# Linear attention, expert MLP and dense MLP on one Trainium2 core: clearing, weight order, late tiles and the last group rearranged

## The chip, the cores and the metric

The kernel runs on one core of one Trainium2 chip. The metric is the device time of one execution in microseconds (us); the median of three executions of the kernel before is 473.36 us (473.33 to 474.61). A difference of 0.3% or less, 1.4 us, can't be told from no change.

## What is computed

The reference, cut to what matters:

```python
def attn(q, k, v, alpha):            # B=2, H=8, S=768, D=48
    for t in range(S):
        state = alpha[:, :, t, :, None] * state + einsum('bhd,bhe->bhde', k[:, :, t], v[:, :, t])
        y[:, :, t] = einsum('bhd,bhde->bhe', q[:, :, t], state)

def moe(x, w_gate, w1, w2, capacity=384):   # x 1536x384, E=8, F=1024
    logits = x @ w_gate; e = argmax(logits); gate_w = softmax(logits)[e]
    # token i goes to the next free slot of expert e, if fewer than capacity are taken
    h = relu(disp @ w1[e]); y = h @ w2[e]
    out[i] = gate_w[i] * y[e, pos[i]]        # 0 where the token was dropped

def mlp(x, w_in, w_out):                     # 384 -> 2048 -> 384
    h = x @ w_in
    return (h * clip(h + 3, 0, 6) / 6) @ w_out

out = mlp(moe(attn(q, k, v, alpha)))
```

## The kernel before

The kernel has three stages, and each engine has its own instruction list, written out by hand; semaphores alone set the order between engines.

**Attention and routing.** The 1536 tokens are 12 tiles of 128. The `for i in range(NT)` loops of the VectorE, ScalarE and TensorE programs (lines 870, 599 and 1112) go through the tiles one by one. For tile `i`, VectorE prepares the decays of tile `i + 3` (`prepare`, five instructions), masks the scores of tile `i + 1` (`mask`) and adds to the state (`update_state`); TensorE computes scores (`front`), state updates (`update`), the carried part (`carry`), the masked part (`mix`), and for the tile before the router's logits (`turn_x`, `logits`); ScalarE copies results out of PSUM. Routing is done in parts, groups of tiles: `PARTS` (line 40) has tiles 0 to 5, 6 to 8, 9, and 10 with 11. For each part, `choose` finds the expert of each token on VectorE, TensorE counts ranks with one-hots (`ranks_before`, `ranks_within`), `exponents` on ScalarE and `weigh` on VectorE give the gates, `place_tokens` the slots. `gate_rows` on ScalarE then scales a token's row by its gate, and GpSimd scatters it to its slot in DRAM with an indirect DMA (line 502). The last part (`LATE`, tiles 10 and 11) is used for the first expert without waiting for that: `gather_first_rows` (line 1147) reads expert 0's rows back from DRAM, transposes them (line 1153, 12 matmuls against the identity), and adds the late tiles by matmuls against one-hots scaled by the gate (line 1159, `to_slots`, six for each late tile).

**Experts.** All weights and inputs are split into a high and a low part (float32r), and three matmuls make a product. `expert(e, r, half)` (line 1203) runs 8 hidden blocks `f` of 9 matmuls and, three blocks behind (`LAG`), 8 output blocks of 9; at `f` = 3, 4 and 6 (`TURN_AT`) it transposes a third of the next expert's rows (line 1166). At `f` = 0, 3, 5 and 7 (`SPLIT_AT`) ScalarE and VectorE split the four pieces of the next expert's weights, raw -> `w_hi` (line 640) -> `w_lo` (line 848). `raw` has one buffer for each piece, so SyncE issues piece `n` of the stage after next when that split is done (`load_piece`, line 331). SyncE's order is: the rows of expert `e + 2`, then its four weight pieces (`during`, line 414). Ahead of the loop stand the loads for expert 2 and one DMA that zeroes the whole output (line 422). GpSimd, once expert 0's rows are turned, clears `x_hi` and `x_lo` (lines 509 and 510), the input of the MLP; ScalarE and VectorE wait for that ahead of expert 1. VectorE works out the offsets of the experts' tokens in that input (lines 933 to 940) between the low parts of expert 0's rows (line 917) and its own part of expert 0.

**MLP.** The weights w_in and w_out are stages 8 and 9. Four groups of three token tiles go through `group` (line 1308): 16 hidden blocks (lines 1174 to 1176) and, three behind, 16 output blocks (lines 1302 to 1304) of nine matmuls of 384 columns. ScalarE copies the three tiles of a group out (line 706), and GpSimd scatters each to its tokens (line 525). A conditional pass (`n_more > 0`) handles experts with more than 232 tokens.

Of the kernel before, what the change touches and what calls it, by code (L numbers as in the profile page):

```python
# [16 lines left out]
def build_program(nc, qk, alpha, v, w_gate, w1, w2, w_in, w_out, out, *, cap):  # L17
# [21 lines left out]

    PARTS = ((0, TPB), (TPB, NT - 3), (NT - 3, NT - 2), (NT - 2, NT))  # L40
    LATE = PARTS[-1]
    NB = E + NG
    FE, FM = F // P, F2 // P
# [11 lines left out]
    with ExitStack() as ctx:  # L55
# [3 lines left out]
        def sem(name):  # L59
            return ctx.enter_context(nc.semaphore(name))  # L60
# [37 lines left out]
        def view(cols):  # L98
            a = arena[0]
            arena[0] += cols  # L100
            assert arena[0] <= ARENA
            return base[:, a:a + cols]
# [13 lines left out]
        rows_at = arena[0]  # L116
        rows = [view(ET * DM) for _ in range(2)]
        routing_at = arena[0]

# [11 lines left out]

        x_late = [base[:, rows_at + (ET + n) * DM:rows_at + (ET + n + 1) * DM] for n in range(2)]
        arena[0] = 0
# [12 lines left out]
        assert arena[0] <= rows_at  # L146
        to_slots = [probs[0][0][:, n * ER:(n + 1) * ER] for n in range(2)]

# [73 lines left out]
        late_gated = sem("late_gated")  # L222
        outputs_zeroed = sem("outputs_zeroed")
        ids_cleared = sem("ids_cleared")
# [110 lines left out]
        def _(sp):  # L335
# [78 lines left out]
            def during(e, r):  # L414

                load_rows(e + 2, r)
                load_stage(e + 2)

            load_rows(2, 0)
            load_stage(2)  # L420

            sp.dma_start(out.rearrange("(c p) d -> p c d", p=P),
                         zrow.rearrange("p (o d) -> p o d", o=1).broadcast_to([P, NT, DM])).then_inc(out_cleared, 16)
            during(1, 1)
            with sp.Fori(1, E // 2 - 1) as t:
# [5 lines left out]
                         allow_slow_non_contiguous=True).then_inc(ids_in, 16)  # L431
            load_stage(E + 1)

            sp.wait_ge(more_end, 1)
# [17 lines left out]
        def _(pool):  # L452
# [54 lines left out]

            pool.wait_ge(rows_turned, KC)
            pool.memset(x_hi[:, :].bitcast(F32), 0.0).then_inc(outputs_zeroed, 1)
            pool.memset(x_lo[:, :].bitcast(F32), 0.0).then_inc(outputs_zeroed, 1)  # L510

# [22 lines left out]
        def _(act):  # L534
# [64 lines left out]
            for i in range(NT):  # L599
                if i == 8:  # L600
                    exponents(0)
                if i == 10:
                    exponents(1)
                if i + 1 < NT:
                    copy_keys(i + 1)
                if i >= 1:
                    copy_xT(i - 1)
                if i + 1 < NT:
                    spread_values(i + 1)
                    scale_state(i + 1)  # L610
                if i == 9:
                    gate_rows(0, (3, 4, 5))
                if i == 10:
                    gate_rows(1, (6,))
                if i == 11:
                    gate_rows(1, (8,))
                    gate_rows(2, (9,))
                if i >= 1:
                    copy_logits(i - 1)
                if 4 <= i < 4 + NPC:  # L620
                    split_first(i - 4)
                copy_x(i)
                if i == 8:
                    gate_rows(0, (0, 1, 2))
                if i == 10:
                    exponents(2)
                    gate_rows(1, (7,))
            copy_xT(NT - 1)
# [41 lines left out]
            act.wait_ge(offsets_ready, 1)  # L670
            act.wait_ge(outputs_zeroed, 2)
            expert(1, 1)
# [53 lines left out]
        def _(dve):  # L726
# [108 lines left out]
            def place_late():  # L835

                a, b = LATE
                dve.wait_ge(late_placed, 1)
                dve.wait_ge(gates_ready, len(PARTS))
                dve.wait_ge(mixed, NT - 1)  # L840
                for i in range(a, b):
                    dve.tensor_scalar(to_slots[i - a], slot_numbers, place[:, i:i + 1], gate[:, i:i + 1],
                                      ALU.is_equal, ALU.mult).then_inc(to_slots_ready, 1)
                dve.tensor_copy(slot[:, a:b], place[:, a:b]).then_inc(slots_ready, 1)
# [25 lines left out]
            for i in range(NT):  # L870
                if i + 1 < NT:
                    mask(i + 1)
                update_state(i)
                if i == 8:
                    place_tokens(0)
                    weigh(0)
                if i == 9:
                    split_lo(0, 0, 0)
                    choose(1)
                if i == 10:  # L880
                    weigh(1)
                    place_tokens(1)
                    choose(2)
                    split_lo(0, 0, 1)
                if i == 11:
                    weigh(2)
                    place_tokens(2)
                    split_lo(0, 0, 2)
                    split_lo(0, 0, 3)
                if i + 3 < NT:  # L890
                    prepare(i + 3)
                if i == 7:
                    choose(0)
            choose(3)
            weigh(3)
# [60 lines left out]
            dve.wait_ge(offsets_ready, 1)  # L956
            dve.wait_ge(outputs_zeroed, 2)
            expert(1, 1)
# [9 lines left out]
            with dve.If(n_more > 0):  # L968
                with dve.Fori(0, n_more) as m:
# [11 lines left out]
                    last.then_inc(more_lo, 1)  # L981

                    e = which(m)
                    at = dve.value_load(offsets[0:1, bass.ds(e, 1)], min_val=0, max_val=NT * P - EN - 1)
                    dve.wait_ge(more_hi, m * 4 + 4)
# [3 lines left out]
                    last.then_inc(more_lo, 1)  # L989
                    dve.wait_ge(more_lo, m * 4 + 4)  # L990
                    for c in range(KC):
# [27 lines left out]
        def _(pe):  # L1019
# [92 lines left out]
            for i in range(NT):  # L1112
                if i + 1 < NT:
                    front(i + 1)
                if i >= 1:
                    turn_x(i - 1)
                if i == 8:
                    pe.wait_ge(const_ready, 4)
                    pe.wait_ge(state_updated, updates_to(i - 1))
                    ranks_within(0)  # L1120
                if i == 9:
                    pe.wait_ge(ranks_read, 1)
                if i == 10:
                    pe.wait_ge(state_updated, updates_to(i - 1))
                    ranks_before(1)
                    ranks_within(1)
                if i == 11:
                    pe.wait_ge(state_updated, updates_to(i - 1))
                    pe.wait_ge(ranks_read, 2)
                    ranks_before(2)  # L1130
                    ranks_within(2)
                update(i)
                carry(i)
                if i >= 1:
                    logits(i - 1)
                mix(i)
# [66 lines left out]
            def expert(e, r, half):  # L1203


                first = isinstance(e, int) and e == 0
                pe.wait_ge(xt_lo_ready, e * KC + KC)
                for f in range(FE):
                    if f % 4 == 0:
                        pe.wait_ge(w_lo_ready, e * NPC + f // 4 + 1)  # L1210
                    hidden(e * FE, f, r)
                    g = f - LAG
                    if g < 0 and not first:
                        outputs(e - 1, FE + g, 1 - r)
                    if g >= 0:
                        if g % 4 == 0:
                            pe.wait_ge(w_lo_ready, e * NPC + 2 + g // 4 + 1)
                        outputs(e, g, r)
                    if half is not None and f in TURN_AT:
                        if f == TURN_AT[0]:  # L1220
                            pe.wait_ge(rows_in[1 - r], half)
                        turn_rows(e + 1, 1 - r, TURN_AT.index(f))
# [13 lines left out]
            with pe.If(n_more > 0):  # L1236
                pe.wait_ge(y_lo_ready, E * KC)
                with pe.Fori(0, n_more) as m:
# [7 lines left out]
                    last.then_inc(more_turned, 1)  # L1246
                    pe.wait_ge(more_lo, m * 4 + 2)
                    for f in range(FE):
# [8 lines left out]
                    last.then_inc(more_hidden, 1)  # L1257
                    pe.wait_ge(more_lo, m * 4 + 3)
                    for c in range(KC):
# [32 lines left out]

            def mlp_outputs(g, f):
                pe.wait_ge(hid_lo_ready, E * FE + g * FM + f + 1)
                o = (f % 4) * DM
                hi, lo = (x[1][:, f // 4, o:o + DM] for x in (w_hi, w_lo))
                for t in range(TT):
                    if f == 0 and g >= 1:
# [9 lines left out]
            def group(g):  # L1308
                for f in range(FM + LAG):
                    if f < FM and not (g == 0 and f < LAG):  # L1310
# [10 lines left out]
            for g in range(NG):  # L1321
                group(g)


# [20 lines left out]
```

## Time and profile before

| | |
|---|---|
| median of three executions | 473.36 us |
| the profiled execution | 473.34 us |
| its span | 471.5 us |
| TensorE busy | 426.0 us |
| VectorE, ScalarE, GpSimd busy | 268.2, 211.1, 61.8 us |
| mean granted TensorE clock | 0.967 |
| attention and routing | 0 to about 97 us |
| gather of expert 0's rows, experts | about 97 to 257 us |
| MLP | about 260 to 463 us |

PE is TensorE, DVE VectorE, ACT ScalarE, POOL GpSimd, SP SyncE. A group of instructions is named by its line, what it writes and what it reads. The number after "x" is a count. The granted clock is the share of TensorE's full clock.

### The profile page before, as it was taken

Reading aid. Unit: us, or ns where it says so; the run is one execution under the profiler, and the core shown is the slowest. Engines: PE = TensorE matmul, PEld = TensorE weight load, DVE = VectorE, ACT = ScalarE, POOL = GpSimd, SP = SyncE. Lnnn points to the kernel's source line nnn. Section 1 sums busy time; section 2 is a strip of 40 time slices with the busy share of each in tenths; the row PEclk is TensorE's granted clock in tenths of the full one; section 3 lists DMA queues with packets and bytes.
Section 4 is the critical chain, followed back from the end, with each engine's and each line's share of the span. In section 5 each row is a group of like instructions: output and inputs, shape, how many; then the busy total and the mean of one; then the engine's idle time right before and its main releaser. Section 6 shows DMA issues by size and latency. Waiting matters only on the chain.

```text
span 471.5 us, 8025 instructions
## 1 busy us (share of the span) xinstructions
PE 426.0 (90%) x3111; PEld 419.6 (89%) x3111; DVE 268.2 (57%) x473; ACT 211.1 (45%) x408; POOL 61.8 (13%) x68
## 2 busy tenths in 40 slices
PE   1899989765998599999998999999999999999992
PEld 1799989655998599999998999999999999999992
DVE  7999998849654466776667365333332433243330
ACT  1255666412652456556565354343333433343331
POOL 8000006538720000000000000020002000020002
PEclk9999999967999599999999999999999999999998
DMA  8999943561699856666575100010000000010001
GB/s 178 297 281 299 297 126 111 193 239 36 134 126 307 299 165 218 221 202 232 153 235 160 60 1 0 1 51 1 0 1 33 18 1 1 0 51 1 0 1 50
DMA packets 37923, 56.36 MB, mean 120 GB/s; under 512 B 4768, under 2 KB 27808, under 8 KB 37888
## 3 DMA queue, kind: packets, MB, share of 16 engines
q1 hardware_dynamic: 35840, 50.95, 37.7%
q0 software_dynamic: 1920, 4.73, 2.6%
q8 instruction: 24, 0.39, 0.4%
q10 hardware_dynamic: 128, 0.20, 0.2%
q14 instruction: 11, 0.09, 0.1%
HBM read 44.06 MB, written 11.81 MB: 118 GB/s over the span
## 4 chain that ended last, share of the span: by engine, by line
PE 70%; DVE 12%; DMA 6%; issue 5%; ACT 3%; SPq 1%; POOL 1%; DVEq 0%; ACTq 0%; POOLq 0%
PE bank L1176 11%; PE bank L1175 11%; PE bank L1174 11%; PE bank L1304 7%; PE bank L1303 7%; PE bank L1302 7%; PE bank L1195 4%; PE bank L1197 4%; PE bank L1196 4%; DMA raw<-w 3%; DVE bwd L743 2%; DVE arena L756 2%; DVE offsets L935 2%; DVE arena L772 1%; DMA arena<-v 1%
## 5 line engine op out<-in xcount | busy, mean ns | idle before, releaser
L848 DVE TENSOR_TENSOR w_lo<-raw,w_hi 128x1536 fp32r<-128x1536 f32 x40 | 70.1, 1757 | 33.5 <-ACT w_hi L640 33.5
L1004 DVE SCALAR_TENSOR_TENSOR arena<-arena,bank 128x384 f32<-128x384 f32 x64 | 35.4, 553 | 83.6 <-ACT arena L712 83.6
L712 ACT ACTIVATE arena<-bank,bias 128x384 f32<-128x384 f32 x64 | 37.0, 578 | 68.5 <-PE bank L1176 68.5
L1174 PE MATMUL bank<-x_hi,w_hi 128*128 128x384 f32 x192 | 64.5, 336 | 2.5 <-issue 2.5
L1195 PE MATMUL bank<-hid_hi,w_hi 128*128 128x232 f32 x192 | 54.4, 283 | 12.7 <-DVE x_lo L925 7.7
L1175 PE MATMUL bank<-x_lo,w_hi 128*128 128x384 f32 x192 | 65.1, 339 | 0.0
L1303 PE MATMUL bank<-w_lo,hid_hi 128*128 128x384 f32 x192 | 64.8, 337 | 0.0
L1176 PE MATMUL bank<-x_hi,w_lo 128*128 128x384 f32 x192 | 64.7, 337 | 0.0
L1304 PE MATMUL bank<-w_hi,hid_lo 128*128 128x384 f32 x192 | 64.7, 337 | 0.0
L1302 PE MATMUL bank<-w_hi,hid_hi 128*128 128x384 f32 x192 | 64.6, 336 | 0.0
L640 ACT ACTIVATE w_hi<-raw 128x1536 fp32r<-128x1536 f32 x36 | 53.2, 1479 | 9.8 <-DMA raw<-w 9.8
L1008 DVE SCALAR_TENSOR_TENSOR hid_lo<-arena,hid_hi 128x384 fp32r<-128x384 f32 x64 | 35.8, 559 | 37.9 <-ACT hid_hi L715 37.9
L1174 PE MATMUL bank<-xt_hi,w_hi 128*128 128x232 f32 x192 | 55.5, 289 | 1.0 <-DVE xt_lo L917 0.9
L1197 PE MATMUL bank<-hid_lo,w_hi 128*128 128x232 f32 x192 | 53.9, 281 | 0.0
L525 POOL DMA_INDIRECT out<-arena,token_at x12 | 11.7, 975 | 321.1 <-ACT arena L706 318.7
L1176 PE MATMUL bank<-xt_hi,w_lo 128*128 128x232 f32 x192 | 53.7, 280 | 0.0
L1196 PE MATMUL bank<-hid_hi,w_lo 128*128 128x232 f32 x192 | 53.7, 280 | 0.0
L1175 PE MATMUL bank<-xt_lo,w_hi 128*128 128x232 f32 x192 | 53.4, 278 | 0.0
L715 ACT ACTIVATE hid_hi<-arena 128x384 fp32r<-128x384 f32 x64 | 33.6, 526 | 43.0 <-DVE arena L1004 39.9
L1195 PEld LDWEIGHTS bank<-hid_hi,w_hi 128*128 128x128 f32 x192 | 38.0, 198 | 13.3 <-DVE x_lo L925 7.5
L1174 PEld LDWEIGHTS bank<-xt_hi,w_hi 128*128 128x128 f32 x192 | 37.6, 196 | 1.6 <-DVE xt_lo L917 1.3
L1197 PEld LDWEIGHTS bank<-hid_lo,w_hi 128*128 128x128 f32 x192 | 37.9, 198 | 0.0
(137 smaller groups left out, 815.2 us busy)
## 6 DMA issues: line engine op xcount, KB each, us to landing
raw<-w SPq DMA_DIRECT2D x32, 768.0 KB, 6.1
slots_x<-arena SPq DMA_DIRECT2D x8, 576.0 KB, 5.7
arena<-qk SPq DMA_DIRECT2D x22, 192.0 KB, 4.4
arena<-slots_x SPq DMA_DIRECT2D x8, 384.0 KB, 4.9
raw<-w_in SPq DMA_DIRECT2D x4, 768.0 KB, 4.5
raw<-w_out SPq DMA_DIRECT2D x4, 768.0 KB, 6.4
arena<-alpha SPq DMA_DIRECT2D x24, 96.0 KB, 3.6
arena<-v SPq DMA_DIRECT2D x12, 192.0 KB, 4.7
```

The lines of the kernel that those rows point to most:

```text
L640: act.activation(w_hi[w][:, n, :], raw[:, n, :], ACT.Copy).then_inc(w_hi_ready, 1)
L712: act.activation(shifted[f % 2], hidden_bank[f % NH][:, 0:BR], ACT.Relu, bias=bias3[:, 0:1]).then_inc(shift_ready, 1)
L848: dve.tensor_tensor(w_lo[w][:, n, :], raw[:, n, :], w_hi[w][:, n, :].bitcast(F32), ALU.subtract)\
L1174: pe.matmul(bank_, hi, hi_in, start=(kc == 0), stop=False)
L1175: pe.matmul(bank_, hi, lo_in, start=False, stop=False)
L1176: return pe.matmul(bank_, lo, hi_in, start=False, stop=(kc == KC - 1))
L1195: pe.matmul(bank_, hi, h_hi, start=(f == 0), stop=False)
L1196: pe.matmul(bank_, lo, h_hi, start=False, stop=False)
L1197: last = pe.matmul(bank_, hi, h_lo, start=False, stop=(f == FE - 1))
L1302: pe.matmul(bank_, h_hi, hi, start=(f == 0), stop=False)
L1303: pe.matmul(bank_, h_hi, lo, start=False, stop=False)
L1304: last = pe.matmul(bank_, h_lo, hi, start=False, stop=(f == FM - 1))
```

## The change

- `PARTS` becomes tiles 0 to 5, 6 and 7, 8, and 9 to 11: three tiles are late. The parts 1 and 2 are handled one tile earlier on VectorE, ScalarE and TensorE, and the first weight split of VectorE (`split_lo(0, 0, 0)`) stands behind `choose(2)`. The late tiles' buffers are put where the attention's `v_apart` and `probs` lie, so `place_late` waits for the last `mix`.
- GpSimd's two clearings and the waits for them go.
- The DMA that zeroes the output moves from ahead of expert 3's rows to behind all weight loads. The rows of expert `e + 2` are loaded ahead of its fourth weight piece in place of ahead of its first.
- In expert 0, TensorE goes through the first three hidden blocks by thirds of the input (`kc` outside), waiting for one third at a time.
- In the last group of the MLP, the last three output blocks are done tile by tile.
- In the conditional pass, the columns behind an expert's own tokens are multiplied with a mask before the addition.

```diff
-    PARTS = ((0, TPB), (TPB, NT - 3), (NT - 3, NT - 2), (NT - 2, NT))
+    PARTS = ((0, TPB), (TPB, NT - 4), (NT - 4, NT - 3), (NT - 3, NT))
     LATE = PARTS[-1]
+    LATE_PART = len(PARTS) - 1
...
+        stays = rows[1][:, 0:MR]
...
-        x_late = [base[:, rows_at + (ET + n) * DM:rows_at + (ET + n + 1) * DM] for n in range(2)]
-        to_slots = [probs[0][0][:, n * ER:(n + 1) * ER] for n in range(2)]
+        to_slots = [probs[n // 2][n % 2][:, 0:ER] for n in range(LATE[1] - LATE[0])]
+        x_late = [v_apart[n // 2][:, n % 2 * DM:(n % 2 + 1) * DM] for n in range(LATE[1] - LATE[0])]
...
@@ SyncE
             def during(e, r):
-                load_rows(e + 2, r)
-                load_stage(e + 2)
-            load_rows(2, 0)
-            load_stage(2)
-            sp.dma_start(out.rearrange("(c p) d -> p c d", p=P),
-                         zrow.rearrange("p (o d) -> p o d", o=1).broadcast_to([P, NT, DM])).then_inc(out_cleared, 16)
+                for n, src in enumerate(stage_source(e + 2)):
+                    if n == NPC - 1:
+                        load_rows(e + 2, r)
+                    load_piece(sp, e + 2, n, src)
+            during(0, 0)
             during(1, 1)
...
             load_stage(E + 1)
+            sp.dma_start(out.rearrange("(c p) d -> p c d", p=P),
+                         zrow.rearrange("p (o d) -> p o d", o=1).broadcast_to([P, NT, DM])).then_inc(out_cleared, 16)
@@ GpSimd
-            pool.wait_ge(rows_turned, KC)
-            pool.memset(x_hi[:, :].bitcast(F32), 0.0).then_inc(outputs_zeroed, 1)
-            pool.memset(x_lo[:, :].bitcast(F32), 0.0).then_inc(outputs_zeroed, 1)
@@ ScalarE
-                if i == 8:
-                    exponents(0)
-                if i == 10:
-                    exponents(1)
+                if i >= 8 and i < 8 + LATE_PART:
+                    exponents(i - 8)
                 if i + 1 < NT:
                     copy_keys(i + 1)
...
                 if i == 10:
-                    gate_rows(1, (6,))
-                if i == 11:
-                    gate_rows(1, (8,))
-                    gate_rows(2, (9,))
+                    gate_rows(2, (8,))
...
                 copy_x(i)
-                if i == 10:
-                    exponents(2)
-                    gate_rows(1, (7,))
+                if i == 9:
+                    gate_rows(1, (6, 7))
...
-            act.wait_ge(outputs_zeroed, 2)
@@ VectorE
-                dve.wait_ge(mixed, NT - 1)
+                dve.wait_ge(mixed, NT)
...
                 if i == 9:
-                    split_lo(0, 0, 0)
-                    choose(1)
-                if i == 10:
                     weigh(1)
                     place_tokens(1)
                     choose(2)
+                    split_lo(0, 0, 0)
+                if i == 10:
+                    weigh(2)
+                    place_tokens(2)
                     split_lo(0, 0, 1)
                 if i == 11:
-                    weigh(2)
-                    place_tokens(2)
                     split_lo(0, 0, 2)
                     split_lo(0, 0, 3)
                 if i + 3 < NT:
                     prepare(i + 3)
                 if i == 7:
                     choose(0)
+                if i == 8:
+                    choose(1)
...
-            dve.wait_ge(outputs_zeroed, 2)
...
+                    dve.tensor_scalar(stays, slot_numbers[:, 0:MR], float(EN), kept[:, bass.ds(e, 1)], ALU.add, ALU.is_ge)
@@ TensorE
-                if i == 9:
-                    pe.wait_ge(ranks_read, 1)
-                if i == 10:
-                    pe.wait_ge(state_updated, updates_to(i - 1))
-                    ranks_before(1)
-                    ranks_within(1)
-                if i == 11:
+                if i in (9, 10):
                     pe.wait_ge(state_updated, updates_to(i - 1))
-                    pe.wait_ge(ranks_read, 2)
-                    ranks_before(2)
-                    ranks_within(2)
+                    pe.wait_ge(ranks_read, i - 8)
+                    ranks_before(i - 8)
+                    ranks_within(i - 8)
...
                 first = isinstance(e, int) and e == 0
-                pe.wait_ge(xt_lo_ready, e * KC + KC)
+                if first:
+                    pe.wait_ge(w_lo_ready, 1)
+                    for kc in range(KC):
+                        pe.wait_ge(xt_lo_ready, kc + 1)
+                        for f in range(LAG):
+                            last = hidden_part(f, kc, 0, xt_hi[0][:, kc * EN:(kc + 1) * EN],
+                                               xt_lo[0][:, kc * EN:(kc + 1) * EN], EN)
+                            if kc == KC - 1:
+                                last.then_inc(hidden_done, 1)
+                else:
+                    pe.wait_ge(xt_lo_ready, e * KC + KC)
...
             def group(g):
-                for f in range(FM + LAG):
+                for f in range(FM + (LAG if g < NG - 1 else 0)):
...
             for g in range(NG):
                 group(g)
+            for t in range(TT):
+                for f in range(FM - LAG, FM):
+                    mlp_outputs(NG - 1, f, (t,))
```

## Rows read from the trace of the kernel before

**Rows 1.** The page, part 1: busy us, share of the span, instructions of each engine.

```profile
PE 426.0 (90%) x3111; PEld 419.6 (89%) x3111; DVE 268.2 (57%) x473; ACT 211.1 (45%) x408; POOL 61.8 (13%) x68
```

**Rows 2.** Waits of PE: engine, line, waited for; us in total, times, longest.

```profile
PE bank L1195 <- DVE x_lo L925: 7.7, 2, 7.3
PE bank L1195 <- DVE hid_lo L945: 5.1, 1, 5.1
PE bank L1153 <- DMA arena<-slots_x: 3.8, 1, 3.8
...
PE bank L1174 <- DVE xt_lo L917: 0.9, 1, 0.9
```

**Rows 3.** Windows: stretch, length; busy of each engine (instructions), PE clock, DMA, GB/s.

```profile
102.20:102.70 0.50, 0.50 (x3) 0.46 (x2) 0.00 (x0) 0.28 (x1) 0.00 (x0) 0.82 0.12 46
114.40:119.20 4.80, 4.78 (x22) 4.80 (x23) 3.17 (x6) 1.91 (x3) 3.78 (x3) 0.50 0.40 128
119.20:130.00 10.80, 10.80 (x97) 10.80 (x97) 7.53 (x11) 6.51 (x10) 8.66 (x8) 0.99 0.62 109
158.90:163.50 4.60, 4.60 (x22) 4.60 (x22) 1.36 (x5) 1.74 (x2) 0.00 (x0) 0.50 0.82 294
```

**Rows 4.** Timeline of POOL and DVE, 104 to 114: start, us, engine, line, instruction.

```profile
104.24 4.53 POOL L509 MEMSET x_hi<- 128x5304 f32 x1 [3.45 <-PE bank L1159]
105.32 7.93 DVE L935 CAST offsets<-arena 1x8 uint32<-1x8 f32 x1
```

**Rows 5.** Timeline of SP at 130, and DMA issues (KB, us to landing).

```profile
130.53 10.81 SPq L396 DMA_DIRECT2D arena<-slots_x  x1
...
out<-arena SPq DMA_DIRECT2D x1, 2304.0 KB, 21.6
```

**Rows 6.** Chain of waits: the first turn of the next rows in experts 3 and 4.

```profile
179.33 0.22 PE bank L1166 x2
...
196.18 0.22 PE bank L1166 x2
```

**Rows 7.** Timeline of DVE, ACT and POOL, 79 to 93.

```profile
79.15 0.18 DVE L800 TENSOR_REDUCE arena<-arena 128x3 f32<-128x24 f32 x1 [1.03 <-ACT arena L576]
80.39 1.35 DVE L772 COPY_PREDICATED arena<-arena,bank 128x512 f32<-128x512 uint32 x2
84.59 0.16 DVE L800 TENSOR_REDUCE arena<-arena 128x1 f32<-128x8 f32 x1
84.85 0.49 ACT L566 ACTIVATE x_rows<-bank 128x384 f32<-128x384 f32 x1 [0.30 <-PE bank L1067]
88.46 3.42 DVE L848 TENSOR_TENSOR w_lo<-raw,w_hi 128x1536 fp32r<-128x1536 f32 x2
88.51 2.55 POOL L502 DMA_INDIRECT slots_x<-x_rows,slot  x1 [0.30 <-ACT x_rows L591]
92.40 0.17 DVE L800 TENSOR_REDUCE arena<-arena 128x2 f32<-128x16 f32 x1 [0.52 <-ACT arena L576]
```

**Rows 8.** Chain of waits, then timeline of PE: scatter, rows back, gather.

```profile
91.36 3.22 DMA slots_x<-x_rows,slot
94.60 3.10 DMA arena<-slots_x
...
97.74 2.93 PE L1153 MATMUL bank<-ident,arena 128*128 128x128 f32 x12 [3.75 <-DMA arena<-slots_x]
100.46 3.71 PE L1159 MATMUL bank<-arena,x_rows 128*128 128x256 f32 x12
```

**Rows 9.** Timeline of DVE, ACT and POOL at the end.

```profile
458.13 0.56 DVE L1008 SCALAR_TENSOR_TENSOR hid_lo<-arena,hid_hi 128x384 fp32r<-128x384 f32 x1 [0.59 <-ACT hid_hi L715]
...
461.66 1.48 ACT L706 ACTIVATE arena<-bank 128x384 f32<-128x384 f32 x3 [3.56 <-PE bank L1304]
462.95 0.97 POOL L525 DMA_INDIRECT out<-arena,token_at  x1 [47.02 <-ACT arena L706]
...
465.51 0.98 POOL L525 DMA_INDIRECT out<-arena,token_at  x1 [0.30 <-issue]
```

More of the change, by code:

```diff
@@ L146, in build_program @@
         assert arena[0] <= rows_at
-        to_slots = [probs[0][0][:, n * ER:(n + 1) * ER] for n in range(2)]
+        assert (LATE[1] - LATE[0]) * ER <= 4 * TW and (LATE[1] - LATE[0]) * DM <= 4 * DM
+        to_slots = [probs[n // 2][n % 2][:, 0:ER] for n in range(LATE[1] - LATE[0])]
+        x_late = [v_apart[n // 2][:, n % 2 * DM:(n % 2 + 1) * DM] for n in range(LATE[1] - LATE[0])]
         a_in = [view(SC + 1) for _ in range(3)]
@@ L222, in build_program @@
         late_gated = sem("late_gated")
-        outputs_zeroed = sem("outputs_zeroed")
         ids_cleared = sem("ids_cleared")
@@ L989, in _ @@
                     last.then_inc(more_lo, 1)
-                    dve.wait_ge(more_lo, m * 4 + 4)
+                    dve.wait_ge(more_lo, m * 5 + 4)
+                    for c in range(KC):
+                        for x, y in ((x_hi, xt_hi[1]), (x_lo, xt_lo[1])):
+                            there = x[:, bass.ds(at + (c * XW + EN), MR)]
+                            last = dve.tensor_tensor(there, there.bitcast(F32), stays, ALU.mult)
+                    last.then_inc(more_lo, 1)
+                    dve.wait_ge(more_lo, m * 5 + 5)
                     for c in range(KC):
@@ L1210, in expert @@
                         pe.wait_ge(w_lo_ready, e * NPC + f // 4 + 1)
-                    hidden(e * FE, f, r)
+                    if not (first and f < LAG):
+                        hidden(e * FE, f, r)
                     g = f - LAG
@@ L1246, in _ @@
                     last.then_inc(more_turned, 1)
-                    pe.wait_ge(more_lo, m * 4 + 2)
+                    pe.wait_ge(more_lo, m * 5 + 2)
                     for f in range(FE):
@@ L1257, in _ @@
                     last.then_inc(more_hidden, 1)
-                    pe.wait_ge(more_lo, m * 4 + 3)
+                    pe.wait_ge(more_lo, m * 5 + 3)
                     for c in range(KC):
@@ L1291, in mlp_hidden, with mlp_outputs @@
                 last.then_inc(hidden_done, 1)
-            def mlp_outputs(g, f):
+            def mlp_outputs(g, f, tiles=range(TT)):
                 pe.wait_ge(hid_lo_ready, E * FE + g * FM + f + 1)
@@ L1296, in mlp_outputs @@
                 hi, lo = (x[1][:, f // 4, o:o + DM] for x in (w_hi, w_lo))
-                for t in range(TT):
+                for t in tiles:
                     if f == 0 and g >= 1:
```

## The prediction

> **What bounds the kernel now.** I began with the page's busy times. TensorE is busy for 426.0 us of 471.5 [rows 1], so the time is its work plus the places where it stands or runs slowly, and busy time elsewhere counts only where TensorE waits for it. Its waits name four such places between attention and MLP [rows 2]: 3.8 us for expert 0's rows, 0.9 us for the last low part of them (L917), 5.1 us in expert 0 (L945), and 7.3 us ahead of expert 2's outputs (L925). In the windows the reader is to see what comes behind each long wait: the granted clock is 0.50, the 1.2 GHz level, for 4.8 us from 114.40 and for 4.6 us from 158.90, with 22 matmuls each; in the 10.80 us at 0.99 there are 97, one for each 0.111 us [rows 3]. At full rate 4.8 us would hold 43, so 21 matmuls or 2.3 us are lost there, and 2.2 us at the other. In the MLP no wait is left, so only its end can give.
>
> **The waits and what makes them.** The 5.1 us: VectorE's offsets copy of 1x8 elements takes 7.93 us, from 105.32 to 113.25, while GpSimd's two clearings run [rows 4]; the first begins at 104.24 and takes 4.53, the second follows with equal size, so they end near 113.3, as the copy does. Expert 0's low parts are queued behind this copy. The 7.3 us: the 2304 KB that zero the output take 21.6 us to land, and SyncE's next DMA, expert 3's rows, is stuck for 10.81 us [rows 5]; expert 3's first weight piece stands behind it, ScalarE and VectorE wait for that piece in the middle of expert 2, and the low part of expert 1's output (L925) is queued behind the split.
>
> **Term 1, the clearings go: 5.1 + 2.3 = 7.4 us.** The memsets and the waits for them add nothing elsewhere: the area is written by each expert's own output. The seven small offset instructions then take some 1.3 us on VectorE, ahead of hid_lo(0), and TensorE has four hidden blocks (36 matmuls, 4.0 us) before it needs that. Bounds: 5.1, if the clock falls all the same, to 8.3.
>
> **Term 2, the zeroing moves behind all weights: 7.3 + 2.2 = 9.5 us.** It is issued behind the last weight piece and has until the first scatter of the MLP, a whole group of about 50 us later, for its 21.6 us; nothing but that scatter waits for it. Of the rows' move, each instruction is one DMA, now between pieces 2 and 3: the rows come two expert blocks `f` earlier than piece 3 and are needed at `f` = 3 of the next expert, six blocks of 2.1 us later; nothing is behind them but piece 3, which is needed at `f` = 7. I cost it at zero; its cover is those 12 us.
>
> **Cross-check of both by the cadence.** Undisturbed experts are 196.18 - 179.33 = 16.85 us apart [rows 6]. The first turn of an expert stands 45 matmuls (5.0 us) behind its first hidden block. TensorE starts expert 0 at 97.74 + 2.72 + 3.71 + 0.89 = 105.06 [rows 2, 8]; undisturbed, expert 3's turn would be at 105.06 + 5.0 + 3 x 16.85 = 160.6 in place of 179.33. That is 18.7 us, 1.8 more than the terms' 16.9. The surplus is small losses around the two stalls; part of it may belong to the first experts for good. I take half: 17.8 us for both, bounds 16.9 and 18.7.
>
> **Term 3, from the last attention tiles to expert 0: 1.6 us.** This has a loss and two gains.
> The loss: choose(1) (79.15 to 80.39, 1.24 us [rows 7]) now stands ahead of mask(10), and TensorE waits for its one-hots before update(9); this delays everything of tile 9 by 1.24. choose(2) needs tile 8's logits and so starts at 79.15 + 1.24 = 80.4; it takes some 1.0 for one tile, and then comes the first weight split, 3.42 / 2 = 1.7, which in the kernel before lay in VectorE's idle time. mask(11) starts near 83.1 in place of 80.39, 2.7 later. From there the chain goes over update(10), ScalarE's state scaling and x(10). x(10)'s copy had 0.30 of idle time before it [rows 7], VectorE's update had about as much, and the rank step of 0.3 leaves tile 11: I estimate that 1.7 remain. Bounds 0 (all of it in idle time) and 2.7. The late choice starts at 92.40 + 1.7 = 94.1.
> The first gain: TensorE is done with the ranks 3.75 ahead of 97.74, at 93.99, which becomes 95.7, and then waits for expert 0's rows. The scatter that releases them is tile 8's in place of tile 9's. Tile 8's row is gated near 86.8; 3.2 us to landing and 3.1 for the rows [rows 8] give 93.1; with the hold of GpSimd spoken of below, 94.2. Both are ahead of 95.7, so the whole 3.8 us wait goes, and the gather starts 2.0 us earlier.
> Against it, the third late tile brings six matmuls of 256 columns. The clock came up at about 102.2, 4.4 us into the gather [rows 3, 8]; twelve such matmuls took from 100.46 to 104.17, of which 1.74 us at half rate, so one costs 0.24 at full rate and 0.47 at half. Now: gather 95.7, its 12 transposes end at 98.4, the clock comes up near 100.1, so 3.6 matmuls slow and 14.4 x 0.24 = 3.4 us fast; the end is at 103.5.
> The second gain: the first three hidden blocks by thirds need only the first third at once; the last third is ready 0.9 us after the gather and is asked for after 18 matmuls (2.0 us). So the 0.9 us wait goes, and expert 0 starts near 103.45, 1.6 us ahead of 105.06. Its low parts come later than before (three blocks end together), but outputs(0) is asked for after 4.0 us, and its input ready after 21 matmuls (2.3 us) and two copies of about 0.4, at 3.2. Bounds of the term: a loss of 1.5, to a gain of 4.0 if the clock never falls.
>
> The Trainium skill, "SBUF — State Buffer", section "Who interferes with whom", says that a VectorE instruction with two SBUF inputs and a GpSimd instruction that reads SBUF exclude each other, the second to issue blocking fully. The row agrees: a scatter issued at 88.51, 0.05 behind a weight split (88.46), took 2.55 us, to 0.9 behind the first split's end [rows 7]. The rule speaks against this change: tile 8's scatter meets the splits at 86 to 91.5. Held for one split it ends near 88.9, which is the 94.2 above.
>
> **Term 4, the last group by tiles: 1.5 us.** The matmuls are the same. The first tile's output is ready 12 matmuls earlier, the second's 6 earlier, so the last tile's scatter need not queue behind two others: it follows the last matmul. Copy start to scatter start is 462.95 - 461.66 = 1.29 us [rows 9], and the last tile is ready 6 matmuls of 0.18 us (0.111 x 384 / 232 columns), 1.1 us, behind the first (461.66), near 462.7. Its scatter starts at 464.0 in place of 465.51. Against it: hid_lo(15), ready at 458.69, is asked for 21 matmuls (3.8 us) before the end at 462.6, at 458.8: 0.1 us of margin. Bounds 1.0 and 1.6.
>
> **Unchanged:** the passage from experts to MLP, where the same two splits are due, and the conditional pass, which no instruction of the trace belongs to: its mask and the added multiplications cost nothing here.
>
> **Sum.** 17.8 + 1.6 + 1.5 = 20.9 us. The profiled execution took 473.34 us, its span 471.5; the median of the runs is 473.36, so no correction: 473.34 - 20.9 = **452.4 us**, the span near 450.6. By the bounds, the terms added linearly give 448.5 to 456.9.
>
> **Rivals.**
> 1. *One of the two big stalls keeps its place under another cause.* For it: without the zeroing, expert 3's piece 0 still follows the late-row wait and a queue that was behind; against it, later experts show no wait with the same loads. The time: 452.4 + 9.5 = 461.9, or 459.8 if it is the one in expert 0. Chance 0.09.
> 2. *The rows become the new wait.* If tile 8's scatter is held through three splits, to 91.5 + 0.9, expert 0's rows come at 97.7 again: 2.0 later, 454.4. If expert 1's rows come late: three late scatters instead of two end near 102.1, land 2.5 later, and the rows come near 107.8 for a turn at 108.5; two microseconds more and TensorE stops, with half clock behind it: 452.4 + 2 + 2.2 = 456.6. Together 0.20.
> 3. *The tail of attention costs nothing, or the clock stays up over the gather.* 1.7 or 2.1 less: 450.5. For it: VectorE had idle time there. Chance 0.12.
> 4. *Slower.* The rows of expert e + 2 now wait behind three weight pieces. Issued at `f` = 5 they have six blocks, 12 us; in rows 5 a DMA in the same queue was stuck for 10.81. If they landed after 16 us in each of experts 2 to 7, each would stop for 4 us and lose 2.2 by the clock: 6 x 6.2 = 37 us, 489 us. It decides against the change from 3.5 us of lost time for each of the six, that is a landing near 13.5 us. Against it: that stuck DMA stood behind 2304 KB, which has gone. Chance 0.02.
>
> **How the numbers follow.** The forecast has 0.57: 450.8 to 454.8. The range reaches from rival 3 to past rival 2's far end: 449.5 to 457.5. A measurement can tell 0.3%, 1.4 us. All but rival 4 is faster by far more: 0.97 faster, 0.01 within 0.3%, 0.02 slower.
>
> **What would show it.** Right: the offsets copy (L935) takes about 0.2 us and no PE wait on L945 is left; SyncE's zeroing stands behind w_out, no L396 over 1 us, no 7 us wait on L925; the first turns of experts 0 to 3 are 17 us apart; the gather starts near 95.7 with no wait for rows, and has 18 matmuls in L1159; the mask of tile 11 starts near 83; the last scatter starts about 1.3 us behind the last copy's start. Wrong: a PE wait over 1 us anywhere between 96 and 240, a clock of 0.50 behind expert 0's start, or a copy of x(11) that is not about 1.7 us later.

## The result and the profile after

The changed kernel was timed in 20 executions beside 20 of the kernel before: median 471.27 us (465.25 to 479.74) against 474.45 us. The ratio is 0.9833, interval [0.9808, 0.9857]. It leaves out executions more than 1.5% above the fastest of their kernel; here these were ten of the 20, at 473.9 to 479.7 us, and the other ten were at 465.3 to 468.6. The forecast was 452.4 us with a range to 457.5. The profiled execution took 468.64 us, the longest of these ten (their median is 466.3), its span 466.7.

The page's busy times, beside [rows 1]:

```profile
PE 428.8 (92%) x3115; PEld 422.3 (90%) x3115; DVE 261.1 (56%) x474; ACT 211.1 (45%) x408; POOL 49.9 (11%) x66
```

TensorE's waits (line, what it waited for; total, times, longest), beside [rows 2]:

```profile
PE bank L1162 <- DMA arena<-slots_x: 10.2, 1, 10.2
...
PE bank L1102 <- DVE onehot L798: 3.5, 3, 1.6
PE bank L1170 <- DVE x_lo L920: 2.4, 1, 2.4
...
PE bank L1149 <- DMA arena<-slots_x: 0.6, 1, 0.6
```

The waits of 5.1 and 7.3 us of [rows 2] are gone, and so is VectorE's 7.93 us copy [rows 4] (it takes 0.16 us). In their place stands one wait of 10.2 us: L1162 turns expert 2's rows in the middle of expert 1. The chain of waits shows what they waited for (start, us, what):

```profile
87.93 5.94 DMA slots_x<-x_rows,slot
93.87 0.02 issue
93.89 3.03 DMA arena<-slots_x
...
110.26 0.22 PE bank L1162 x2
...
118.01 19.73 DMA arena<-slots_x
137.74 0.04 issue
137.79 0.69 PE bank L1162 x2
```

Expert 2's rows, issued at 118.01, took 19.73 us to land. The timelines of SyncE and GpSimd show that time; a count of x4 is four issues with what lies between them:

```profile
118.01 0.51 SPq L398 DMA_DIRECT2D arena<-slots_x  x1
121.84 26.36 SPq L333 DMA_DIRECT2D raw<-w  x4
...
108.60 0.97 POOL L516 DMA_INDIRECT token_ids<-token,position  x1 [5.64 <-issue]
...
126.33 0.97 POOL L516 DMA_INDIRECT token_ids<-token,position  x1 [0.30 <-issue]
```

GpSimd issues the 12 scatters of token numbers (L516) from 108.6 to 127.3, each of 128 elements of 4 bytes. The windows have the columns of [rows 3]; the last three are the granted clock, the DMA engines' busy share and GB/s. From 120 to 124 and from 130 to 137.8 us they show DMA engines that are busy and move little; in the second of these stretches TensorE stands, and its clock is at the 1.2 GHz level for the 4.7 us behind the wait:

```profile
74.00:76.00 2.00, 0.83 (x6) 0.84 (x7) 1.86 (x10) 0.77 (x3) 1.56 (x2) 0.85 0.27 98
76.00:78.00 2.00, 2.00 (x11) 2.00 (x11) 1.28 (x4) 0.78 (x3) 0.97 (x1) 0.50 0.47 166
...
120.00:124.00 4.00, 4.00 (x38) 4.00 (x37) 3.93 (x4) 2.14 (x4) 3.39 (x3) 1.00 0.73 48
...
130.00:137.80 7.80, 0.01 (x1) 0.01 (x1) 0.00 (x0) 0.00 (x0) 0.00 (x0) 0.50 0.91 77
137.80:142.50 4.70, 4.70 (x23) 4.70 (x23) 2.47 (x3) 2.10 (x3) 0.00 (x0) 0.50 0.45 168
...
257.00:259.00 2.00, 2.00 (x8) 2.00 (x7) 0.00 (x0) 0.00 (x0) 0.00 (x0) 0.50 1.07 405
```

The last row lies behind the wait of 2.4 us between experts and MLP (2.5 us before). There the clock fell this time; in the trace of before it did not.

**Where 471.5 became 466.7.** Expert 0 starts at 104.88 in place of 105.06: -0.2. The experts take 147.9 us in place of 152.6: -4.7. From there to TensorE's end it is 206.6 in place of 205.0, by the half clock at 257: +1.6. From TensorE's end to the end of the span it is 7.4 in place of 8.9: -1.5. The sum is -4.8. The start of expert 0 in the timeline of PE:

```profile
99.68 5.54 PE L1155 MATMUL bank<-arena,x_rows 128*128 128x256 f32 x18
104.88 0.46 PE L1170 MATMUL bank<-xt_hi,w_hi 128*128 128x232 f32 x1
```

### The profile page after: what moved, and what is told of

Read it like the earlier page. It is cut to its first block, busy times and chain, and to the rows that moved or that the text cites. A ratio compares the mean times of both kernels' runs of the same rounds, so it can differ in the third digit from the quotient of the medians.

```text
span 466.7 us, 8032 instructions
## 1 busy us (share of the span) xinstructions
PE 428.8 (92%) x3115; PEld 422.3 (90%) x3115; DVE 261.1 (56%) x474; ACT 211.1 (45%) x408; POOL 49.9 (11%) x66
## 4 chain that ended last, share of the span: by engine, by line
PE 80%; DMA 7%; DVE 7%; issue 2%; ACT 2%; POOL 1%; SPq 0%; DVEq 0%; POOLq 0%; ACTq 0%
PE bank L1171 12%; PE bank L1172 12%; PE bank L1170 12%; PE bank L1312 7%; PE bank L1311 7%; PE bank L1310 7%; DMA arena<-slots_x 5%; PE bank L1191 4%; PE bank L1193 4%; PE bank L1192 4%; PE bank L1069 2%; PE bank L1028 2%; PE bank L1047 2%; DVE bwd L737 1%; DVE arena L750 1%
## 5 line engine op out<-in xcount | busy, mean ns | idle before, releaser
L655 ACT ACTIVATE hid_hi<-bank 128x232 fp32r<-128x232 f32 x64 | 23.1, 364 | 35.2 <-PE bank L1172 35.0
L1170 PEld LDWEIGHTS bank<-x_hi,w_hi 128*128 128x128 f32 x192 | 36.5, 190 | 2.6 <-issue 2.6
```

The costliest lines, as they stand in the source:

```text
L1170: pe.matmul(bank_, hi, hi_in, start=(kc == 0), stop=False)
```

## Experiments

There are three theories. A: the scatters of token numbers hold the DMA engines from about 108 to 138 us, and what is issued in that time lands late. B: the rows are late because they stand behind three weight pieces. C, for the ten long executions: the new wait of TensorE at 74 us (1.6 us, for the one-hots of tiles 6 and 7) lets its clock fall in the attention. Medians of before beside them were 474.3 (e1 to e4), 474.8 (e5 to e8) and 473.6 us (e9, e10).

**e1_rows2_early**

```diff
             load_rows(1, 1)
+            load_rows(2, 0)
             def during(e, r):
                 for n, src in enumerate(stage_source(e + 2)):
-                    if n == NPC - 1:
+                    if n == NPC - 1 and not (isinstance(e, int) and e == 0):
```

> The changed kernel, with expert 2's rows loaded right behind expert 1's, ahead of expert 2's weight pieces, as the kernel before had it. Theory A (the 12 scatters of token numbers, each of 128 elements of 4 bytes, hold the DMA engines from about 108 to 138 us, and what is issued in that time lands late): these rows are issued near 105, ahead of the scatters, and land within 5 us; the 10.2 us wait of TensorE on L1162 and the half clock behind it (2.2 us) go, so the profiled time falls from 468.6 to about 456, unless a weight piece becomes late in the same stretch. Theory B (the rows are late because they stand behind three weight pieces in SyncE's order, whatever GpSimd does): the same 456. This run sets the price of the wait; the next one tells the theories apart.

Measured: 455.12 us in the profiled execution, others 454.7, 458.6 and 466.1; ratio 0.9634 [0.9558, 0.971]. The wait of 10.2 us is 0.4:

```profile
PE bank L1163 <- DMA arena<-slots_x: 0.4, 1, 0.4
```

One DMA, issued at 105 in place of 118, goes with 13.5 us between the profiled executions: 9.8 of the wait, 2.1 of the half clock behind it (23 matmuls in 4.7 us, which hold 42 at full rate), and 1.6 because the clock did not fall at 257 in this one. Between the medians of the shorter executions (466.3 and 455.1) it is 11.2 us.

**e2_ids_late**

```diff
             pool.wait_ge(position_ready, 1)
+            pool.wait_ge(raw_in[3], (E + 2) * 16)
...
-            sp.wait_ge(ids_scattered, NT * 16)
-            sp.dma_start(token_at[:, :], token_ids.rearrange("(c p) o -> p (c o)", p=P), ...)
             load_stage(E + 1)
...
+            sp.wait_ge(ids_scattered, NT * 16)
+            sp.dma_start(token_at[:, :], token_ids.rearrange("(c p) o -> p (c o)", p=P), ...)
             sp.wait_ge(more_end, 1)
```

> The changed kernel, with the 12 scatters of token numbers (and the load of their result) moved to behind the last weight load, some 145 us later, where the DMA engines have nothing to do; the order of rows and weights is that of the changed kernel. Theory A: expert 2's rows, issued near 118, land within 6 us, no wait on L1162 is left, 468.6 falls to about 456. Theory B: the rows stay late by about 10 us and the time stays at 466 to 469.

Measured: 463.99 to 466.44 us in all four, ratio 0.9828 [0.9779, 0.9878]. By the time alone this looks like theory B. The trace says otherwise: no wait on expert 2's rows is left. They stand behind the same three pieces, issued at 128.1, and none of the eight loads of rows takes over 5.2 us. The first line is the changed kernel's, the second e2's:

```profile
DMA to landing us min/median/max: 3.0/4.8/19.7
```

```profile
DMA to landing us min/median/max: 2.9/4.9/5.2
```

The DMA engines move 250 to 309 GB/s behind 124 us, where the changed kernel's moved 48 from 120 to 124. Theory A holds, B falls. The time was lost elsewhere, in the attention:

```profile
76.00:78.00 2.00, 1.68 (x13) 1.69 (x13) 1.87 (x7) 1.49 (x4) 1.64 (x2) 0.79 0.49 181
78.00:106.00 28.00, 26.49 (x143) 25.38 (x143) 12.58 (x33) 9.24 (x25) 6.93 (x7) 0.50 0.52 178
124.00:128.00 4.00, 4.00 (x38) 4.00 (x38) 3.16 (x7) 2.48 (x4) 0.00 (x0) 1.00 0.86 309
128.00:136.00 8.00, 8.00 (x74) 8.00 (x73) 5.36 (x8) 4.89 (x9) 0.00 (x0) 1.00 0.82 250
```

Behind the 1.6 us wait at 74.7 us the clock falls and stays at half for over 28 us, where the changed kernel's trace has it for some 3 us (75.4 to 78.7). The ranks of the last part are counted at 108.1 in place of 95.8: 12 us. The wait alone does not do it: e1 has the same wait, in its trace the clock stays at 1.00, and the ranks are counted at 94.7. A line of e1's waits and its windows:

```profile
PE bank L1103 <- DVE onehot L799: 3.5, 3, 1.6
```

```profile
66.00:76.00 10.00, 7.81 (x84) 7.28 (x83) 9.46 (x32) 5.34 (x15) 2.05 (x2) 1.00 0.13 40
76.00:90.00 14.00, 13.07 (x129) 12.68 (x129) 12.03 (x35) 8.74 (x26) 7.64 (x8) 1.00 0.50 166
```

**e3_before_zero_late** (on the kernel before)

```diff
             load_stage(2)
-            sp.dma_start(out..., zrow...).then_inc(out_cleared, 16)
             during(1, 1)
...
             load_stage(E + 1)
+            sp.dma_start(out..., zrow...).then_inc(out_cleared, 16)
```

> The kernel before with one edit: the zeroing of the output (2304 KB) stands behind all weight loads. The prediction's own theory (the zeroing makes expert 3's first weight piece late): the 7.3 us wait on L925 and its half clock (2.2) go, 473.4 falls to about 464. Theory A (the scatters of token numbers hold the DMA engines until some 5 us behind the last of them, 133.6): most of the wait stays, since piece 0 of expert 3 is issued into the same stretch; the time is 468 to 473.

**e4_before_ids_late** (on the kernel before, with e2's diff alone)

> The kernel before with one edit: the 12 scatters of token numbers moved to behind the last weight load; the zeroing stays at its place. Theory A: the zeroing then takes about 6 us of the DMA engines (2304 KB at some 400 GB/s) in place of 21.6, SyncE is not stuck for 10.8 us, and the 7.3 us wait goes or falls under 1 us: about 464. The prediction's own theory: the zeroing still stands ahead of the weight piece, the wait stays near 7 us, 473.

Measured: e3 464.79 to 470.68 us, median 466.2, ratio 0.9859 [0.9785, 0.9934]; e4 457.29 to 465.26 us, median 464.0, ratio 0.9717 [0.9617, 0.9818]. The 7.3 us wait of [rows 2] in each:

```profile
PE bank L1195 <- DVE x_lo L925: 2.3, 1, 2.3
```

```profile
PE bank L1197 <- DVE x_lo L927: 0.8, 1, 0.8
```

and the zeroing in e4, which took 21.6 us to land [rows 5]:

```profile
out<-arena SPq DMA_DIRECT2D x1, 2304.0 KB, 11.9
```

Either edit removes most of the wait. Neither the prediction's theory nor A has it alone: the scatters, issued from 114.8 to 133.6, and the 2304 KB, under way from 130 to 152, made it together, and nearly half of the zeroing's 21.6 us went with the scatters.

**e5_ranks_later**

```diff
-                if i >= 8 and i < 8 + LATE_PART:
+                if i in (8, 10):
                     exponents(i - 8)
...
                     spread_values(i + 1)
+                    if i == 9:
+                        exponents(1)
                     scale_state(i + 1)
@@ TensorE
+                if i == 10:
+                    pe.wait_ge(state_updated, updates_to(i - 1))
+                    pe.wait_ge(ranks_read, 1)
+                    ranks_before(1)
+                    ranks_within(1)
                 if i + 1 < NT:
                     front(i + 1)
...
-                if i in (9, 10):
+                if i == 9:
+                    pe.wait_ge(ranks_read, 1)
+                if i == 10:
```

> e1_rows2_early, and in it TensorE counts the ranks of tiles 6 and 7 one tile later (ahead of the scores of tile 11), and ScalarE takes their exponents behind the copy of the values, so that TensorE no longer stands 1.6 us at 74 us waiting for one-hots. Theory C: that wait is what lets TensorE's clock fall to half in the attention (for 4 us in the changed kernel's trace, from 76 to 103 us in e2_ids_late's), and so makes the runs some 10 us longer in part of the executions. Then the granted clock is 1.00 from 66 to 92 us, all runs are at 452 to 456 us, and none over 460. Rival D: the clock falls by the thin work of these tiles whatever this wait does; then the profile or some of the runs still show it, at 463 to 467.

Measured: 453.36 to 461.74 us, ratio 0.9618 [0.9558, 0.9678]. The clock is 1.00 from 66 to 90 us in the profiled execution (454.42 us). But four of six executions are at 459.5 to 461.7, where I expected all at 452 to 456. Their mean clock is 0.963 to 0.966 in place of 0.989, so it fell somewhere in them too; no profile of one of these was taken, so where is open, and rival D (the thin work lets it fall, whatever this wait does) is not excluded. Executions at 463 or more, as in e1 and e2, did not come.

**e6_ids_late_too** (e5 with e2's diff)

> e5_ranks_later, and the 12 scatters of token numbers behind the last weight load as in e2_ids_late. If the scatters hold the DMA engines but no wait of TensorE is left that stands on a DMA in that stretch (e1_rows2_early had none over 0.4 us), this brings nothing: the time of e5_ranks_later within 1.5 us. If the clogged engines still cost something, it is 2 us or more faster.

Measured: 454.03 to 460.47 us, ratio 0.9658 [0.9618, 0.9699]: nothing gained over e5, as expected where no wait stands on a DMA of that stretch; again four of six are at 458.8 to 460.5. The profiled executions can't tell what e5's edit of the ranks does: the last part's ranks are counted at 96.5 in e6 and at 108.1 in e2, but at 94.7 in e1, whose attention is the same as e2's. What speaks for the edit is the count of executions: none of the twelve of e5 and e6 is over 462 us, while one of e1's four and all four of e2's are at 464 or more, and half of the changed kernel's are some 10 us above its others.

**e7_two_late_tiles** (on e1; with it, each line of the routing on VectorE, ScalarE and TensorE is that of the kernel before)

```diff
-    PARTS = ((0, TPB), (TPB, NT - 4), (NT - 4, NT - 3), (NT - 3, NT))
+    PARTS = ((0, TPB), (TPB, NT - 3), (NT - 3, NT - 2), (NT - 2, NT))
```

> e1_rows2_early with the parts, the late tiles and the order of the routing of the kernel before (tiles 0-5, 6-8, 9, two late tiles); all other edits of the change in it. If the three late tiles and earlier parts bring what the prediction's term 3 said for them (the waits for rows gone, the gather 2.0 us earlier, less 0.4 to 2 for six more matmuls), this run is about 1 us slower than e1_rows2_early's fast runs. If they cost, by the wait for one-hots, the later tiles and the longer gather, it is 1 us or more faster, at 452 to 454 us, and no run is at 463 or more.

Measured: 451.57 to 457.97 us, median 453.77, ratio 0.9583 [0.9541, 0.9625], the fastest of all versions. Its gather, and that of e1 (three late tiles), in the timeline of PE:

```profile
96.82 2.93 PE L1157 MATMUL bank<-ident,arena 128*128 128x128 f32 x12 [3.50 <-DMA arena<-slots_x]
99.53 3.33 PE L1163 MATMUL bank<-arena,x_rows 128*128 128x256 f32 x12
102.51 0.46 PE L1178 MATMUL bank<-xt_hi,w_hi 128*128 128x232 f32 x1
```

```profile
97.13 2.93 PE L1150 MATMUL bank<-ident,arena 128*128 128x128 f32 x12 [1.91 <-DMA arena<-slots_x]
99.85 5.35 PE L1156 MATMUL bank<-arena,x_rows 128*128 128x256 f32 x18
104.86 0.46 PE L1171 MATMUL bank<-xt_hi,w_hi 128*128 128x232 f32 x1
```

With three late tiles TensorE waits 1.9 in place of 3.5 us for the rows, but it comes there later; the gather starts 0.3 us later and takes 2.0 us more. Expert 0 starts 2.35 us later than with two.

**e8_before_no_clearing** (on the kernel before)

```diff
-            pool.wait_ge(rows_turned, KC)
-            pool.memset(x_hi[:, :].bitcast(F32), 0.0).then_inc(outputs_zeroed, 1)
-            pool.memset(x_lo[:, :].bitcast(F32), 0.0).then_inc(outputs_zeroed, 1)
...
-            act.wait_ge(outputs_zeroed, 2)
...
-            dve.wait_ge(outputs_zeroed, 2)
```

> The kernel before with one edit: GpSimd's two clearings and the waits for them gone (with the mask of the conditional pass that replaces them). The prediction: 5.1 us of wait and 2.3 us by the clock go, 474.3 falls to about 467. Rival: the wait behind expert 2 is set by when the DMA engines are free, not by the experts' time; with expert 0 ahead by 7 us, and the scatters of token numbers 7 us earlier as well, it should not grow, but if it does by as much, the time stays at 472 to 474.

Measured: 467.49 to 469.81 us, median 468.2, ratio 0.9872 [0.9846, 0.9899]. Between the profiled executions 5.3 us are gained, by the medians 6.6, of the predicted 7.4. The wait on the low part of expert 1's output (L925 before, here L920) grew from 7.3 to 8.0 us, and a second one for a low part of rows, 1.4 us, joined:

```profile
PE bank L1196 <- DVE x_lo L920: 8.0, 1, 8.0
...
PE bank L1175 <- DVE xt_lo L912: 2.3, 2, 1.4
```

So of what was gained in expert 0, about 2 us were given back in the experts behind it.

**e9_stall_added** (on e7)

```diff
                 if i == 9:
                     pe.wait_ge(ranks_read, 1)
+                    pe.wait_ge(masked, 11)
```

> e7_two_late_tiles with one wait added: at tile 9, ahead of its state update, TensorE waits for the mask of tile 10, which ends near 75.1; by that kernel's trace TensorE is there at 72.9, so it stands for 2.1 us, about where the changed kernel stands 1.6 us for one-hots. Behind it on TensorE are the update, carry, logits and mix of tile 9; VectorE waits for the update. Theory C (such a wait is what lets the clock fall to half in the attention): the granted clock between 75 and 80 us falls to 0.5 in the profile or the runs spread to some 6 to 12 us above the fastest, with a median of 458 to 464. Rival D (the clock falls for other reasons): the clock stays 1.00 up to 92 us, and the median is that of e7_two_late_tiles, 453.8, plus 0 to 2 us.

Measured: 455.1 to 459.8 us in four executions, 465.6 and 467.1 in two, median 457.7, just under the 458 to 464 expected. The profiled execution is the one at 465.6. Its windows, and those of e7 without the wait:

```profile
74.00:78.00 4.00, 1.89 (x17) 1.71 (x16) 2.71 (x6) 1.52 (x4) 3.07 (x3) 1.00 0.26 98
78.00:106.00 28.00, 26.51 (x153) 25.34 (x152) 13.62 (x39) 9.85 (x27) 8.00 (x7) 0.50 0.41 136
```

```profile
78.00:84.00 6.00, 5.44 (x58) 5.14 (x54) 4.78 (x22) 3.61 (x12) 3.26 (x4) 1.00 0.72 264
84.00:92.00 8.00, 6.00 (x64) 5.46 (x63) 6.80 (x18) 3.95 (x10) 5.91 (x4) 1.00 0.56 172
```

A wait of 2.1 us, added to a kernel that had none there, gives e2's picture: half rate from 78 to over 106 us, and some 11 us on the time, in part of the executions. Over all profiled executions: of the four kernels with such a wait between 73 and 77 us, the clock falls behind it in three (changed, e2, e9) and not in e1; of the eight without it, none has a clock under 1.00 from 66 to 90 us. So such a wait can bring the fall on, in some executions and not in others. With one profile for each kernel this is good evidence for theory C, not proof.

It is not the only way to a long execution: e10, which has no such wait and was timed beside e9, has one at 462.92 us (mean clock 0.964), and the kernel before, timed beside both, has one at 480.48 (0.953, its others 470.9 to 476.6). That the wait makes the changed kernel's ten long executions is likely (they are 10 us longer at a lower mean clock) and not shown, since none of them was profiled.

**e10_two_late_ids_late** (e7 with e2's diff)

> e7_two_late_tiles with the 12 scatters of token numbers behind the last weight load. In e7_two_late_tiles' trace TensorE stands 1.0 us on L1199 and 0.5 on L1170 between 125 and 145 us, both behind loads; with the DMA engines free these go, 0.5 to 1.5 us of gain, 452 to 453.5 us. If the gain is nil, the waits there were not the scatters'.

Measured: 453.43 to 454.47 us in five, 462.92 in one, median 454.3; ratio 0.9586 [0.9545, 0.9628]. The waits between 125 and 145 us are gone, and the median is that of e7 within 0.5 us. The gain expected was not there; its clock fell once more in another place, behind the experts (0.83 from 236 to 245 us), where e7's did not.

## Why the prediction was wrong

**The step that failed: the rows' move, "I cost it at zero; its cover is those 12 us" (term 2).** It priced the move without a landing time; the median of the eight loads of rows, 4.8 us, would have fitted. But once, for expert 2, these rows are issued into the scatters of token numbers, and took 19.7 us. The kernel before issued them at 103, ahead of the scatters. The wait of 10.2 and its half clock of 2.1 us are 12.3 of the 17.8 us that terms 1 and 2 forecast; e1 undoes this one move and comes to 455.1 us, and e2, which moves the scatters away, has no wait on the rows. The cover, too, was smaller than 12 us: TensorE asked for the rows at 127.5, 9.5 behind their issue, which came 7.7 us (nearly four blocks) behind expert 0's turn at `f` = 3 (110.26), not at `f` = 5. Rival 4 named this outcome with another cause, the weight pieces ahead (theory B, which fell), with those 12 us as the threshold, and priced it for six experts; it struck one, and I had given it 0.02.

**The size of terms 1 and 2.** Without the late rows the experts take 135.9 us in e1 and 136.5 in e7, in place of 152.6: 16.7 and 16.0 us for the 17.8 forecast. The plain sum of the terms, 16.9, was nearer than the cadence's 18.7, whose surplus did not appear.

**Term 2, the cause of the 7.3 us.** Half right: e3 has most of its gain (8.1 us between medians, 9.5 forecast), but e4 gets 10.3 by moving the scatters alone. The row that I read as the price of the zeroing, 21.6 us to landing, was inflated by them: away from them it is 11.2 (changed kernel) to 12.4 us (e1), and 15.2 in e2, where both stand behind the last weights. I had written that row down and not asked why 2304 KB should take 21.6 us, which is some 109 GB/s, when a stretch of [rows 3] moves 294.

**Term 1, the clearings.** Right in mechanism: the offsets copy is short and the wait on L945 gone. Its size was 5.3 to 6.6 us (e8) for 7.4, some being returned in the next experts.

**Term 3, attention to expert 0.** The loss was forecast well. In the timeline of DVE after, the mask of tile 11 starts at 83.41 (83.1 forecast), the last choice at 94.68 (94.1):

```profile
83.41 1.35 DVE L766 COPY_PREDICATED arena<-arena,bank 128x512 f32<-128x512 uint32 x2
...
94.68 0.18 DVE L794 TENSOR_REDUCE arena<-arena 128x3 f32<-128x24 f32 x1 [2.89 <-ACT arena L577]
```

What failed is the wait for expert 0's rows, which was to go whole. Tile 8's row was gated at 87.1 (86.8 forecast), but its scatter starts 0.85 us behind that, at 87.93, a step that the forecast left out, and took 5.9 us to land in place of 3.2. So the rows were there at 96.9, where 94.2 was forecast with GpSimd's hold. Why the scatter landed late is open. The hold itself was small: the scatter took 1.37 us on GpSimd in place of 0.97. TensorE came at 96.3 (95.7 forecast), and 0.6 us of wait remained. The gather took 7.9 us, 7.8 forecast. The sum is a gain of 0.2 for a forecast gain of 1.6. Missed altogether: TensorE's 1.6 us wait for the one-hots of tiles 6 and 7. I put its delay on the chain, but not what a standing TensorE does to its clock, though [rows 3] showed what a fall costs. The start by thirds of the input did what was said: no wait of 0.9 us is left.

**Term 4, the last group by tiles.** Right: the last scatter starts 1.29 us behind its own tile's copy, where [rows 9] have 3.85 us from the first copy to the third scatter, and 1.5 us are gained for 1.5 forecast. The timelines of ACT and POOL after:

```profile
459.38 0.49 ACT L700 ACTIVATE arena<-bank 128x384 f32<-128x384 f32 x1 [1.07 <-PE bank L1312]
...
460.67 0.97 POOL L526 DMA_INDIRECT out<-arena,token_at  x1 [0.59 <-issue]
```

**Unforeseen, +1.6 us:** the clock fell behind the unchanged wait between experts and MLP, as it had not in the trace of before.

**The bounds.** The lower one should read 449.0 (473.34 less 18.7, 4.0 and 1.6), not 448.5; nothing hangs on it.

With the rows early and two late tiles, e7 has terms 1, 2 and 4 and the start by thirds. Their forecasts, 17.8, 1.5 and 0.9 us, would give 453.1; its profiled execution took 453.4, its median is 453.8. Part of this agreement is luck: the experts give 16.0 of the 17.8, and expert 0 starts 2.5 us earlier in place of 0.9.

## What to carry to other kernels

A load that is moved in a queue is moved in time: look at what all queues, the slow small ones above all, have in flight at its new place, not at the load's usual landing time. A row that shows a transfer far under the rate of its neighbours is a question, not a price. And where TensorE is nearly always busy, a new wait of 1.6 us can cost more than itself: it can bring down the clock over a long stretch of thin work behind it, in some executions and not in others, so compare several executions before a version is called better.

## What the runs showed of the hardware

Twelve scatters of 128 elements of 4 bytes move 6 KB in all. In the changed kernel they were issued from 108.6 to 127.3 us, and from 120 to 124 and from 130 to 137.8 us the DMA engines were 73 to 91% busy at 48 to 77 GB/s; between these stretches they also moved more, 359 GB/s from 127.5 to 130. With the scatters elsewhere the loads of rows landed within 5.2 us (e2) in place of 19.7, and the zeroing in 11.9 us (e4) in place of 21.6. Why 6 KB hold the engines so long no run shows.

TensorE's clock, once it fell to the 1.2 GHz level at 75 to 78 us, came back after some 3 us in one execution (the changed kernel's profile) and stayed down to 106 us and beyond in others (e2, e9), over nearly the same instructions: 26.5 us of 28 busy by the trace. Behind the stalls in the expert stage, with dense matmuls, it came back within 4.8 us each time ([rows 3], and the changed kernel's row from 137.8 us).
